# Attention and two gated MLPs on one core: the front before the first down product re-ordered, its column sums folded on VectorE

## The reference, cut to what matters

```
qn = q / (norm(q, axis=1) + 1e-6)          # q, k, v: 6016 x 256, norms over the 6016 rows, one per column
kn = k / (norm(k, axis=1) + 1e-6)
a  = softmax(kn.T @ qn / tau)              # 256 x 256, over rows
x  = v @ a                                 # 6016 x 256
h = x @ w_in1;  x = (h * sigmoid(1.702 * h)) @ w_out1      # 256 -> 2048 -> 256
h = x @ w_in2;  x = where(h > 0, h, exp(min(h, 0)) - 1) @ w_out2
```

## Time and profile before

| | us |
|---|---|
| median of 3 runs | 1057.63 (1056.87 to 1057.79) |
| the profiled execution | 1056.41 |
| its span, first to last instruction | 1054.7 |
| PE busy in the span | 1038.2 (98%) |
| ACT, DVE, POOL busy | 765.5, 760.6, 24.4 |

### The profile page before, as it was taken

The page is one execution under the profiler, slowest core; times in us unless marked ns, Lnnn a source line. Parts: engine busy times, 40 slices in busy tenths (PEclk is TensorE's granted clock), DMA queues, the critical chain, the costliest instruction groups (busy, mean ns, idle before and its releaser), DMA issues.

```text
span 1054.7 us, 14140 instructions
## 1 busy us (share of the span) xinstructions
PE 1038.2 (98%) x4682; PEld 868.8 (82%) x4682; DVE 760.6 (72%) x1236; ACT 765.5 (73%) x1373; POOL 24.4 (2%) x22
## 2 busy tenths in 40 slices
PE   9989999999999999999998999999999999999996
PEld 8978888888888888888986887887887888888896
DVE  6488866556665655655878788888888887788775
ACT  7686766556566656556779888788888788788874
POOL 3220000000000000000000000000000000000000
PEclk9899999999999999999999999999999999999998
DMA  9913003003002102003113001101201100110112
GB/s 340 288 21 80 1 1 80 1 1 71 10 1 60 18 1 58 1 1 120 41 48 108 1 1 51 30 1 41 41 1 41 25 16 23 33 20 1 21 21 35
DMA packets 107512, 46.26 MB, mean 44 GB/s; under 512 B 90928, under 2 KB 98352, under 8 KB 106800
## 3 DMA queue, kind: packets, MB, share of 16 engines
q1 hardware_dynamic: 107440, 45.36, 16.0%
HBM read 33.03 MB, written 12.32 MB: 43 GB/s over the span
## 4 chain that ended last, share of the span: by engine, by line
PE 92%; ACT 4%; DVE 2%; issue 2%; DVEq 0%; ACTq 0%; POOL 0%; POOLq 0%
PE bank L974 29%; PE bank L976 29%; PE bank L975 29%; PE bank L984 3%; ACT xo L639 1%; ACT act_out L572 1%; PE bank L999 1%; ACT blk_hi L496 1%; DVE gated L807 1%; PE bank L981 0%; ACT g_hi L590 0%; DVE s_sum L840 0%; ACT u L532 0%; DVE g_lo L820 0%; PE bank L1076 0%
## 5 line engine op out<-in xcount | busy, mean ns | idle before, releaser
L974 PE MATMUL bank<-g_hi,w_dn_hi 128*128 128x512 f32 (+1 forms) x768 | 296.2, 386 | 0.8 <-DVE g_lo L820 0.8
L976 PE MATMUL bank<-g_hi,w_dn_lo 128*128 128x512 f32 (+1 forms) x768 | 295.8, 385 | 0.0
L975 PE MATMUL bank<-g_lo,w_dn_hi 128*128 128x512 f32 (+1 forms) x768 | 295.7, 385 | 0.0
L820 DVE TENSOR_TENSOR g_lo<-gated,g_hi 128x512 fp32r<-128x512 f32 (+1 forms) x384 | 259.8, 676 | 48.3 <-ACT g_hi L590 42.4
L974 PE MATMUL bank<-blk_hi,w_up_hi 128*128 128x512 f32 (+1 forms) x672 | 261.9, 390 | 6.6 <-DVE w_up_lo L780 2.3
L975 PE MATMUL bank<-blk_lo,w_up_hi 128*128 128x512 f32 (+1 forms) x672 | 259.2, 386 | 0.0
L976 PE MATMUL bank<-blk_hi,w_up_lo 128*128 128x512 f32 (+1 forms) x672 | 259.2, 386 | 0.0
L590 ACT CAST g_hi<-gated 128x512 fp32r<-128x512 f32 (+1 forms) x288 | 175.7, 610 | 21.7 <-DVE gated L807 21.7
L974 PEld LDWEIGHTS bank<-g_hi,w_dn_hi 128*128 128x128 f32 x768 | 144.2, 188 | 28.9 <-DVE g_lo L820 1.9
L976 PEld LDWEIGHTS bank<-g_hi,w_dn_lo 128*128 128x128 f32 x768 | 144.2, 188 | 27.0
L975 PEld LDWEIGHTS bank<-g_lo,w_dn_hi 128*128 128x128 f32 x768 | 144.2, 188 | 26.8
(11 more groups left out here) (121 smaller groups left out, 776.4 us busy)
## 6 DMA issues: line engine op xcount, KB each, us to landing
x_scratch<-xo SPq DMA_DIRECT2D x10, 512.0 KB, 3.1
raw<-x_scratch SPq DMA_DIRECT2D x5, 1024.0 KB, 4.8
out_dram<-blocks SPq DMA_DIRECT2D x40, 128.0 KB, 2.7
qk<-in_q_dram SPq DMA_DIRECT2D x12, 384.0 KB, 9.5
qk<-in_k_dram SPq DMA_DIRECT2D x12, 384.0 KB, 10.4
blocks<-in_v_dram SPq DMA_DIRECT2D x36, 128.0 KB, 3.4
stage<-in_moe_w_in_dram SPq DMA_DIRECT2D x8, 512.0 KB, 7.7
stage<-in_moe_w_out_dram SPq DMA_DIRECT2D x8, 512.0 KB, 4.6
```

The costliest lines, as they stand in the source:

```text
L820: nc.vector.tensor_tensor(g[1][:, x, 0:w], gated[:, n % 2, 0:w], g[0][:, x, 0:w].bitcast(F32), ALU.subtract).then_inc(c_glo, 1)
L974: nc.tensor.matmul(out_ps, w_hi, x_hi, start=start, stop=False, skip_group_check=goes_on)
L975: nc.tensor.matmul(out_ps, w_hi, x_lo, start=False, stop=False, skip_group_check=goes_on)
L976: return nc.tensor.matmul(out_ps, w_lo, x_hi, start=False, stop=stop, skip_group_check=goes_on)
```

## The change

- Groups: fourteen groups of three steps, then 2, 1, 1, 1 (before: 2, 1, 1, 2, twelve of three, then 2, 1, 1, 1). Fourteen steps are split in place of thirteen, and POOL makes all their low parts; 11 idle turns in place of 14.
- Column sums: before, PE multiplied three lanes and three last squares by ones, 24 matmuls. After, ACT copies one lane to `sumsq`, DVE adds the two other lanes and the three last squares (which now lie in PSUM) one after the other, and PE does four matmuls. They stand ahead of both steps of group `LANES - 1`, where they stood between its two steps.
- ACT squares groups 13, 14, 15, copies the lane, squares 16 and 17, and only then casts the high parts of groups 13, 15 and 16.
- w_in1: DVE makes two of the four low parts, between the reciprocals and the row of norms; POOL makes the other two in halves. Two high parts are cast ahead of the root, the third ahead of the exponentials, the fourth behind the second transposed exponential. Three quarters are loaded ahead of v, where two were.
- Unit 0: new orders on ACT, DVE and PE.

```diff
-    G_STEPS = [2, 1, 1, 2] + [3] * 12 + [2, 1, 1, 1]
+    G_STEPS = [3] * 14 + [2, 1, 1, 1]
...
-    SPLIT_GROUPS = list(range(5, 16)) + [LANES, LANES + 1]
-    BY_GPSIMD = 11
+    SPLIT_GROUPS = list(range(2, 14)) + [LANES, LANES + 1]
...
-        sq_last = [x.rearrange("p (a c) -> p a c", a=2) for x in (gated[:, 0, :], gated[:, 1, :], h22[:, :])]
+        sq_last = [banks[i][:].rearrange("p (a c) -> p a c", a=2) for i in (3, 5, 4)]
...
-        IDLE_TURNS = 14
+        IDLE_TURNS = 11
+        W1_BY_VECTOR = 2
...
-            load_w_in1(0)
-            load_w_in1(1)
+            for fb in range(FB - 1):
+                load_w_in1(fb)
...
-            load_w_in1(2)
-            load_w_in1(3)
+            load_w_in1(FB - 1)
...
-            for fb in range(FB):
+            for fb in range(W1_BY_VECTOR, FB):
                 pool.wait_ge(c_w1hi, fb + 1)
-                nc.gpsimd.tensor_tensor(wi1(1, fb), stage1[:, fb, :].rearrange("p (k f) -> p k f", k=KC),
-                                        wi1(0, fb).bitcast(F32), ALU.subtract).then_inc(c_w1lo, 1)
+                for j in range(KC):
+                    nc.gpsimd.tensor_tensor(wi1(1, fb)[:, j, :], stage1[:, fb, j * BANK:(j + 1) * BANK],
+                                            wi1(0, fb)[:, j, :].bitcast(F32), ALU.subtract).then_inc(c_w1late, 1)
...
-            squared = 0
-            for n in range(NG):
-                if n == LANES:
-                    act.wait_ge(c_sum, SUM_ZERO + LANES)
-                    nc.scalar.copy(lanes[:, :, :, :], sums[:, :, :, :]).then_inc(c_lanes, 1)
+            for n in range(LANES - 2):
                 if n in SPLIT_GROUPS:
                     split_hi(n)
-                while squared < SQUARES_UP_TO[n]:
-                    square(squared)
-                    squared += 1
+                square(n)
+            for n in range(LANES - 2, LANES + 1):
+                square(n)
+
+            act.wait_ge(c_sum, SUM_ZERO + LANES - 1)
+            nc.scalar.copy(sumsq[:, :, :], sums[:, GROUP - 1, :, :]).then_inc(c_fold, 1)
+            for n in range(LANES + 1, NG):
+                square(n)
+            for n in (LANES - 2, LANES, LANES + 1):
+                split_hi(n)
...
+            w1_hi(0)
+            w1_hi(1)
             act.wait_ge(c_norm, 1)
             nc.scalar.activation(roots, col_sums, ACT.Sqrt).then_inc(c_root, 1)
             nc.scalar.activation(small[:, 1:2], small[:, 1:2], ACT.Exp)
-            w1_hi(0)
-            w1_hi(1)
+            w1_hi(2)
...
             et_hi(0)
-            w1_hi(2)
+            et_hi(1)
             sum_of_row()
-            et_hi(1)
+            w1_hi(FB - 1)
...
-            aw_raw(0)
             block_hi(0, X11)
             block_hi(0, X21)
+            aw_raw(0)
             aw_raw(1)
-            w1_hi(3)
             up_hi(0, 0)
...
+            dve.wait_ge(c_sum, SUM_ZERO + LANES)
+            for lane in reversed(range(GROUP - 1)):
+                dve.wait_ge(c_fold, GROUP - 1 - lane)
+                nc.vector.tensor_tensor(sumsq[:, :, :], sumsq[:, :, :], sums[:, lane, :, :], ALU.add).then_inc(c_fold, 1)
+            for n in range(LANES, NG):
+                dve.wait_ge(c_sq, n + 1)
+                dve.wait_ge(c_fold, GROUP + n - LANES)
+                nc.vector.tensor_tensor(sumsq[:, :, :], sumsq[:, :, :], sq_last[n - LANES], ALU.add).then_inc(c_fold, 1)
...
+            for fb in range(W1_BY_VECTOR):
+                dve.wait_ge(c_w1hi, fb + 1)
+                nc.vector.tensor_tensor(wi1(1, fb), stage1[:, fb, :].rearrange("p (k f) -> p k f", k=KC),
+                                        wi1(0, fb).bitcast(F32), ALU.subtract).then_inc(c_w1lo, 1)
             dve.wait_ge(c_norm, 2)
...
             et_lo(0)
+            et_lo(1)
+            copy_v(0)
+            t_of(0, T1)
             inverse_of_row()
-            copy_v(0)
-            et_lo(1)
-            t_of(0, T1)
             copy_v(1)
+            block_lo(0, X11)
             t_of(0, T2)
-            block_lo(0, X11)
             block_lo(0, X21)
             up_sums(0)
             up_lo(0, 0)
...
             def norms():
-                for x in range(NG - LANES):
-                    pe.wait_ge(c_sq, LANES + x + 1)
-                    column_sums(sq_last[x], x == 0, False)
-                pe.wait_ge(c_lanes, 1)
-                for lane in range(GROUP):
-                    mm = column_sums(lanes[:, lane, :, :], False, lane == GROUP - 1)
+                pe.wait_ge(c_fold, GROUP + NG - LANES)
+                for x in range(2 * KC):
+                    mm = nc.tensor.matmul(col_sums[:, x:x + 1], sumsq[:, x // KC, (x % KC) * P:(x % KC + 1) * P], ones[:, 0:1],
+                                          start=True, stop=True)
                 mm.then_inc(c_norm, 1)
...
             a_w(4)
             product1(0)
+            product2(0)
+            product1(1)
             a_w(5)
-            product2(0)
             product6(0)
+            product5(0)
+            product7(0)
             a_w(6)
-            product7(0)
-            product5(0)
-            product1(1)
+            a_w(7)
             product2(1)
-            a_w(7)
             product4(0)
             product3(0)
```

More of the change, by code:

```diff
@@ L111, in attention_and_two_mlps @@
         with ExitStack() as early:
-            lanes = sb(early, "lanes", [P, GROUP, 2, C])
+            sumsq = sb(early, "sumsq", [P, 2, C])
         u1 = sb(ctx, "u1", [P, T])
@@ L184, in attention_and_two_mlps @@
         c_w1lo = sem("c_w1lo")
+        c_w1late = sem("c_w1late")
         c_aw = sem("c_aw")
@@ L408, in _ @@
                                     pattern=[[-1, P]], channel_multiplier=1).then_inc(c_const, 1)
-            for i, n in enumerate(SPLIT_GROUPS[:BY_GPSIMD]):
+            for i, n in enumerate(SPLIT_GROUPS):
                 pool.wait_ge(c_qkhi, i + 1)
@@ L608, in _ @@
             up_hi(0, 2)
+            dn_hi(0)
             copy_u1(0)
             aw_raw(3)
-            dn_hi(0)
+            aw_raw(4)
             block_hi(0, T3)
+            block_hi(0, T4)
+            copy_u2(0)
             up_hi(1, 0)
+            aw_raw(5)
+            copy_u3(0)
+            block_hi(0, X22)
             up_hi(1, 1)
-            copy_u2(0)
             gelu(0, H11)
-            block_hi(0, T4)
             g_hi(0, H11)
[L619 to L622, removed]
             aw_raw(6)
@@ L708, in _ @@
                 nc.vector.tensor_tensor(part, part, sq[n % 2][:, :, 0:G_STEPS[n], :], ALU.add).then_inc(c_sum, 1)
[L710 to L713, removed]
+            assert G_STEPS[LANES - 2:] == [GROUP, GROUP - 1] + [1] * (NG - LANES)
+            dve.wait_ge(c_sum, SUM_ZERO + LANES)
[6 more added lines that the diff above has]
+                nc.vector.tensor_tensor(sumsq[:, :, :], sumsq[:, :, :], sq_last[n - LANES], ALU.add).then_inc(c_fold, 1)
             steps_done = [0]
@@ L875, in _ @@
             block_lo(0, T2)
+            up_lo(0, 1)
+            t_of(0, T3)
+            up_lo(0, 2)
+            t_of(0, T4)
             block_lo(0, T1)
-            t_of(0, T3)
-            up_lo(0, 1)
-            up_lo(0, 2)
             sum11_of(0)
-            t_of(0, T4)
             block_lo(0, T3)
@@ L884, in _ @@
             up_lo(1, 0)
-            up_sums(1)
+            dn_lo(0, 1)
             block_lo(0, T4)
             sum22_of(0)
-            g_lo(0, H11)
             block_lo(0, X22)
             up_lo(1, 1)
-            dn_lo(0, 1)
+            g_lo(0, H11)
+            up_sums(1)
             def y_of(p, tile):
@@ L988, in split_step, with norms @@
                 part = SPLIT_GROUPS.index(n)
-                if part < BY_GPSIMD:
-                    pe.wait_ge(c_qklo, part + 1)
-                else:
-                    pe.wait_ge(c_qklast, part - BY_GPSIMD + 1)
+                pe.wait_ge(c_qklo, part + 1)
                 hi, lo, rows = qk_hi[:, part % PARTS, :, :], qk_lo[:, part % PARTS, :, :], slice(i * P, (i + 1) * P)
                 return three_pass(s_ps[i], hi[:, 1, rows], lo[:, 1, rows], hi[:, 0, :], lo[:, 0, :], False, False, True)
-            def column_sums(of, start, stop):
+            def norms():
+                pe.wait_ge(c_fold, GROUP + NG - LANES)
                 for x in range(2 * KC):
-                    mm = nc.tensor.matmul(col_sums[:, x:x + 1], of[:, x // KC, (x % KC) * P:(x % KC + 1) * P], ones[:, 0:1],
-                                          start=start and x == 0, stop=stop, skip_group_check=True)
-                return mm
-            def norms():
-                for x in range(NG - LANES):
-                    pe.wait_ge(c_sq, LANES + x + 1)
-                    column_sums(sq_last[x], x == 0, False)
-                pe.wait_ge(c_lanes, 1)
-                for lane in range(GROUP):
-                    mm = column_sums(lanes[:, lane, :, :], False, lane == GROUP - 1)
```

(12 more changed lines are left out.)

4 lines of the change are left out of this document (1 added, 3 removed).

## The result

| | before | after |
|---|---|---|
| median, us | 1057.66 (1056.87 to 1057.79, 4 runs) | 1048.55 (1047.43 to 1051.2, 4 runs) |
| the profiled execution | 1056.41 | 1047.43 |

The ratio is 0.9919 (95%: 0.99 to 0.9939). A second set of runs of the same changed kernel gave 1046.32 against 1056.31, 0.9909 (0.9894 to 0.9924): 9 to 10 us. The forecast was 12.2 us less, 1045.4; its range of 1044.0 to 1049.4 held in both sets, its narrow range of 1045.2 to 1046.9 only in the second. In that second set the kernel before took from 1053.8 to 1058.4 us, the shorter times at a higher mean clock (0.996 near 1054, 0.993 near 1056.6); its trace, of 1056.41 us, is one of the longer kind, so the half-clock stretches of the earlier trace rows need not stand in every execution.

The account below looks back on a forecast made before the run. PE's own work bounds 78.65 to 1048 us, so the front's length decides; gains 0.67 + 0.15 + 5.55 + 1.8 + 4.0 = 12.2 us give 1057.6 - 12.2 = 1045.4, range 1044.0 to 1049.4.

Parts of the forecast that it names:

- narrow range: Forecast's own range, chance 0.61: 18.3 or 20.0 us in the last stage, from first `a_w` to first `down`.
- step 42, which lands at 4.95 + 39 x 0.26 MB at 403 GB/s = 30.3: Loads of q and k ahead of the norms: DVE's sums stand at 35.5, leaving the fold 0.5 to 0.8 us slack.
- the gain of 0.67 + 0.15 us at the start: Start of PE's scores: 0.67 us from three fewer idle turns, less 0.15 for one more split step.
- The lower rate that the prediction also tried: Loads at some 358 GB/s: step 42 lands near 33 us, PE waits 2 us at the norms, total 1047.5.
- rival (a): Late loads at the norms: PE waits 2.0 us, perhaps 1.7 more for clock; 1047.4 to 1049.1, chance 0.18.
- Column products and clock: At the norms, four products replace 24, gaining 5.55 us; full clock through the last scores gains 1.8.
- DVE's low parts of w_in1: Between reciprocals and row of norms: at most 1.38 us, hidden by the scores' second half; without it 0.5 cost.
- First `a_w` to first `down`: Last stage of the front: 18.5 us instead of 22.46, gain 4.0, of which 1.7 is clock.
- Rival (b): Ahead of product 1: PE again waits 2.35 us instead of 0.5 and the clock falls, 1.7; 1049.0, chance 0.16.
- the other direction: Near 43.6 us, POOL's first half would delay DVE's low parts of w_in1, making the sum 1.2 us more.
- (c): Clock falls at the norms and stays down until unit 1: half clock adds about 24 us, 1069; chance 0.03.
- (d): At the norms the wait only moves: fold ends when the 24 products did, clock falls as before; 1056.5, chance 0.02.

## Why the prediction's range held and its gain was 2 to 3 us too large

| term | forecast, us | profile after |
|---|---|---|
| first score; column products begin | 5.35; 39.8 | 5.15; 41.83 |
| step 42 lands | 30.3 | 32.8 |
| sums complete behind it; fold | 5.2; 3.5 to 3.8 | 5.1; 3.8 |
| column products to softmax | 45.7 - 39.8 = 5.9 | 5.43 |
| softmax | 2.31 | 2.09 |
| first `a_w` to first `down`; wait at product 1 | 18.5; 0.2 to 0.6 | 18.62; 0.40 |
| first `down` | 66.5 | 67.97 |

**The step that failed** is "step 42, which lands at 4.95 + 39 x 0.26 MB at 403 GB/s = 30.3". It landed at 32.79, 2.5 us later, and the gain of 0.67 + 0.15 us at the start became a loss of 1.0. The first three steps landed at 5.10, 0.15 later than reckoned. From there to the landing of step 42 the table by stage of the changed kernel has:

```profile
5.10:32.79 27.69, 27.38 (x151) 24.48 (x150) 21.20 (x12) 24.53 (x24) 14.10 (x11) 1.00 1.02 390
```

Two things were mis-sized. The rate was 390 GB/s over this stretch, though 401 from 10 to 30 us: the 10.2 MB of 39 steps take 26.2 us at 390 instead of 25.4 at 403, which is 0.8 us. And the bytes do not land in the order of the groups: 390 GB/s for 27.69 us are 10.8 MB, of which 0.6 MB belong to other transfers and take 1.5 us. With the 0.15 this is the whole error. The rows show where it came in: 1.2 us at the second group (3.16 us behind the first, where 0.79 MB at 403 GB/s are 1.95), and about 1.0 at 22.94. The trace shows one such transfer: the q of the group behind, 0.26 MB, landed at 32.09, ahead of the k that ends step 42. With the loads behind q and k held back it was no different:

```profile
0.00:33.10 33.10, 32.04 (x172) 29.22 (x173) 22.65 (x15) 26.01 (x26) 14.79 (x18) 1.00 0.96 363
```

These are 12.0 MB by the landing of step 42, where 42 steps are 11.0, so there the bytes ahead were those of later q and k. The Trainium skill, DMA: Bandwidth & Descriptors, section Why a DMA increments its semaphore by 16 and not by 1, says that a DMA's engines finish independently and that only the last one's completion means that all has landed; the bytes ahead agree with it. What decides how many they are is not shown: fewer groups under way lost the rate. Why a k falls a further microsecond behind its q from about 20 us on stays open. The lower rate that the prediction also tried put the landing near 33 us; that this came near is luck, for the bytes moved faster than that.

What hangs on the landing is shown. In the eight traces in which PE waits for the fold, the column products began 9.0 to 9.1 us behind the landing of step 42, while that landing lay between 32.57 us (fourteen idle turns) and 34.56 (few groups under way).

So rival (a) came about, without its fall of the clock. From the profiled 1056.41 us its sum gives 1056.4 - 12.2 + 2.0 = 1046.2, and the profiled execution took 1047.43, of which 1.1 us were the slow matmuls at its end; counted from the median of before, the same sum is 1047.4, for medians of 1048.55 and 1046.32. The wait of 2.0 us that it puts at the norms was spread: 0.31 us at the second group, 0.39 behind POOL and 0.73 behind the fold are the 1.43 that PE was idle until 41.83, and the rest shows in no wait of its own. Since the loads set this stage, three idle turns more or less, the old groups and an earlier first score changed nothing measurable.

**Column products and clock** (forecast 5.55 and 1.8, 7.35 together) held, and a little more: with the step that moved counted on both sides it is 7.6. The experiments from both sides agree that this is the larger part of the change: the fold alone brought 6.2 us, and without it 5.9 were lost. That four products keep the clock full is not a rule of these traces: of ten with four products it fell behind them in two, with the loads held back and with few groups under way, after waits of 0.56 and 0.75 us in the first of these, where 0.39 and 0.73 were followed by full clock in the changed kernel.

**DVE's low parts of w_in1** were costed at nothing, with the second half of the scores as cover. PE waited 0.20 us for the exponentials: nearly hidden, as forecast. With the old place of the products, which takes one step from the cover, PE waited 1.05 us there; with no low parts on DVE the stretch to the first `a_w` was 0.5 us shorter.

**First `a_w` to first `down`** (forecast gain 4.0, measured 3.84) held with its mechanism: pair of adds 0.75 instead of 2.96, wait at product 1 0.40 instead of 2.35, clock full. Rival (b) did not come. The Trainium skill's rule in SBUF — State Buffer, Who interferes with whom, that of two such instructions on the shared port the second waits, agrees with the 2.94 us beside POOL's 2.64. Where DVE's low parts of w_in1 had started first (43.97 to 46.33), it was POOL that lost: its first half, from 45.60 on, took 1.87 us of the 3.10 below, the second 1.27, so the 1.2 us of the other direction did not come (GpSimd's rows of the changed kernel):

```profile
45.60 3.10 POOL L417 TENSOR_TENSOR w_dn_lo<-stage,w_dn_hi 128x512 fp32r<-128x512 f32 x2 [3.05 <-ACT w_dn_hi L458]
51.12 2.55 POOL L417 TENSOR_TENSOR w_dn_lo<-stage,w_dn_hi 128x512 fp32r<-128x512 f32 x2 [2.43 <-ACT w_dn_hi L458]
```

From the first `down` to the end of PE's last matmul it had been 968.2 us before; the changed kernel took 969.9 in the first profile and 968.7 in the second. The forecast took this part as unchanged.

Rivals (c) and (d) did not come: the clock was at 1.00 from 4.16 us to 1041.81, and the fold ended at 41.69, not where the 24 products had ended.

## What to carry to other kernels

When many transfers are under way, reckon the landing of the n-th with some of the bytes issued behind it and with the rate of the whole stretch, or read it from the trace; the best rate alone gave 2.5 us too early here. A run of 24 one-column matmuls cost its own time and, in the traces here, the clock of the work behind it, so sums that feed such matmuls are worth folding on an engine with slack. Where two engines slowed each other, taking the two instructions apart in time was worth more than re-ordering everything around them: 2 us against 0.3 in the traces.

## What was not expected of the hardware

- The full clock is first on record at 4.16 us in one profile of the changed kernel and at 6.29 in the other (the clock column shows 1.00 ahead of it too, for want of a record); the same idle turns ended at 5.15 and 5.92.
- A wait of 2.35 us of PE was followed by half clock before, and one of 2.59 in the same place was not when only the fold was changed.
- Matmuls of 448 columns came every 203 ns on the mean in most executions, and every 206 to 207 in the last part of one.
- VectorE's `tensor_scalar` on 128x4 and 128x2 took 0.75 and 0.99 us while GpSimd ran, each until GpSimd's instruction ended, and 0.17 and 0.23 otherwise.
